# Filling half of the first expert's slots from the token groups already routed, and computing their products among the routing of the last group

## The chip, the cores and the metric

The kernel runs on 1 core of one Trainium2 chip. The metric is the time of one execution on the device, in microseconds (us), as the median over runs.

## What is computed

A linear attention with a decay per head, a gated MLP, and a mixture of experts in which each token goes to one expert:

```python
def reference(**kwargs):
    attn_out = _attn_ref(**attn_kwargs)                    # 2 x 8 heads x 768 x 64
    x = np.ascontiguousarray(attn_out.transpose(0, 2, 1, 3)).reshape(B * S, H * D)   # 1536 x 512
    x = _moe_ref(x=x, **moe_kwargs)       # silu(x @ w_gate) * (x @ w_val) @ w_out, d_ff 1536
    return _moe2_ref(x=x, **moe2_kwargs)

def _moe2_ref(x, w_gate, w1, w2):         # N 1536, D 512, E 8, F 1024
    logits = x @ w_gate
    expert_idx = np.argmax(logits, axis=1)
    probs = softmax(logits)
    for e in range(E):
        mask = expert_idx == e
        h = np.maximum(x[mask] @ w1[e], 0.0)
        out[mask] = gate_w[mask, None] * (h @ w2[e])
```

## The kernel before

Every product of the MLP and of the experts is made from float32 operands that are split in a high and a low part (fp32r), with three terms (`split_terms`): high times high, high times low, low times high. ScalarE (ACT) makes the high parts by a copy, VectorE (DVE) the low parts by a subtraction (helper `low`, L976 to L979).

**Attention**, 12 chunks of 128 tokens (`scores` L537, `from_state` L550, `to_state` L559, `within` L575), in plain f32.

**MLP**, three groups (`NG`) of 512 tokens, each with 12 units f (`NF1`) of 128 hidden columns. For each unit TensorE makes gate and val (`gate_val` L603, 24 products of 512 columns) and later the out products (`out_product` L618, 12 products, which wait for `hl`). gate_val of unit f+1 stands ahead of out_product of unit f. ACT and DVE have for each unit a function `unit` (L858, L1097): sigmoid, product, split of the next unit's weights, then `hid`, `hh`, `hl`. `first_half` holds units 0 to 5 and, spread among them, the routing of the group before; `second_half` units 6 to 11. In the last group's second half the weights of expert 0 are also loaded by GpSimd (POOL, `load_chunk` L420, eight halves of four pieces through `stage[2]`) and split (`split_first_expert`).

**Routing** of a group: the output is evacuated from PSUM in high and low part (`evacuate`), `logit_product` (L629, 8 products of 512 columns), DVE's `copy_logits`, `turn_logits` (four small transposes), `rows` (L651, four transposes for each of four tiles, which bring tokens onto partitions), ACT's `rows_out`, a store of each tile to `x2_rows` in DRAM. DVE's `choose` (L1130) finds the expert of each token, TensorE's `ranks` (L663) its rank among the tokens of that expert from the counts in `before`, `find_slots` and `place_tokens` (L1149, L1168) turn it to a slot, and `count_choices` adds the group to `before`. For the last group all this stands behind the MLP, and then a table: 12 small products (L722) give for each slot its token, DVE writes it as `idx`, and one product of `before` with ones counts the tokens of each expert, from which `passes` follows (one pass takes up to `CAP` = 256 tokens of each expert; slots go in token order). Two bursts of products that nothing reads, `keep_clock` (L658, 8 and 18 of them), stand in this stretch:

```python
            ranks(NG - 1)
            pe.wait_ge(ewl_ready, 1)
            keep_clock(8)
            for t in range(NT):          # the table, 12 products
            ...
            keep_clock(18)
            pe.wait_ge(idx_ready, 1)
            pe.wait_ge(slots_ready, 1)
```

**Experts.** POOL gathers the 256 rows of an expert by indirect DMA in two tiles `gx[0]`, `gx[1]` (`gather` L448), after it has waited for the stores of all rows. `transpose_rows` (L730) turns them (two times four transposes), ACT and DVE split them (`tokens`). Each expert then has 8 steps f: `hidden` (L739, 12 products of 256 columns, weights 128x128), ACT's Relu to `ehh` and DVE's low part `ehl`, `outward` (L752, 2 tiles x 3 products of 512 columns, which wait for `ehl`). Hidden f+1 stands ahead of outward f. Meanwhile the weights of the next expert are split, its rows transposed at f = 4, and its softmax factors made. `ys` is scaled by the gate and scattered by POOL. `read_passes` (L273) loads the number of passes to a register on each engine, ahead of expert 0. Experts 0 to 5 are a loop of two, then 6, then `last_expert`.

The order of the work on each engine is the order in which it is written. Buffers of the MLP and of the experts share memory (`region2`), as do routing tables and `stage[3]` (`region0`), so that e.g. the second expert's weights may be written only when the MLP's operands have been read.

Of the kernel before, what the change touches and what calls it, by code (L numbers as in the profile page):

```python
# [65 lines left out]
def bass_linear_attention_mlp_moe(nc, attn_in, lam_rows, mlp_w, router_w, expert_w, out):  # L66
    ctx = ExitStack()
    with ctx:
# [17 lines left out]
        idx_now = [sb(f"idx_now{i}", [P, 1], I32) for i in range(4)]  # L86
        gate_now = [sb(f"gate_now{i}", [P, 2]) for i in range(2)]
# [18 lines left out]
        mosti = sb("mosti", [P, 1], I32, region0)  # L106
        region0.close()
# [46 lines left out]
        lt = sb("lt", [2 * E, GT], F32, region2)  # L154
        region2.close()
# [77 lines left out]
        gate_ready_x = sem("gate_ready_x")  # L233
        gx_read = sem("gx_read")

# [32 lines left out]
        TOKEN_BANK, COUNT_BANK = 4, 5  # L268
# [18 lines left out]
        def _(sp):  # L287
# [46 lines left out]
            sp.wait_ge(gx_read, 4)  # L334
# [13 lines left out]
        def _(pool):  # L348
# [78 lines left out]
            with pool.Fori(1, PIECES) as q:  # L427
                for j in range(2):
                    pool.wait_ge(ewl_ready, q * 2 + (j - 1))
                    load_chunk(q, j)  # L430

            pool.wait_ge(rows_psum, NT)
            for i in range(2):
                nc.gpsimd.memset(gx[i][:, :], 0.0).then_inc(gx_read, 1)
            for t in range(GTT):
                pool.wait_ge(x2_stored[t], 16 * NG)

            def copy_idx(x, par):
                for i in range(2):
                    nc.gpsimd.tensor_copy(idx_now[2 * par + i][:, :],  # L440
                                          idx[:, bass.ds(x * 2 + i, 1)]).then_inc(now_ready, 1)

            def fetch(dst, src, at, done):
                nc.gpsimd.indirect_dma_start(
                    out=dst[:, :], out_offset=None, in_=src, in_offset=bass.IndirectOffsetOnAxis(ap=at, axis=0),
                    bounds_check=N - 1, oob_is_err=False).then_inc(done, 16)

            def gather(x):  # L448
                pool.wait_ge(gx_read, x * 2 + 2)
# [16 lines left out]
            def first_pass():  # L466
                gather(0)
                nc.gpsimd.memset(idx_now[0][:, :], 0).then_inc(now_ready, 2 * E)
# [8 lines left out]
            def gather_by_copy(x, par):  # L477

                pool.wait_ge(gx_read, x * 2 + 2)
# [3 lines left out]
                pool.wait_ge(now_ready, x * 2 + 2)  # L483
                for i in range(2):
                    fetch(gx[i], x2_rows, idx_now[2 * par + i][:, 0:1], gx_landed[i])

            def scatter_by_copy(x, par):
                for i, ready in ((0, y0_ready), (1, y1_ready)):
                    pool.wait_ge(idx_ready, 1)
                    pool.wait_ge(ready, x + 1)  # L490
                    put(i, idx_now[2 * par + i][:, 0:1])
# [28 lines left out]
            def ahead():  # L520
                pool.wait_ge(now_ready, 2 * E)
# [12 lines left out]
        def _(pe):  # L534
# [123 lines left out]
            def keep_clock(count):  # L658

                for _ in range(count):  # L660
                    mm(bank[:, ROWS_BANK, :], ewh0[:, 0, 0:P], ewh0[:, 0, KD * P:], start=True, stop=True)

# [29 lines left out]

            def second_half(g, end=False):
# [17 lines left out]
            second_half(NG - 1, end=True)  # L711
            logit_product(NG - 1)
            before_turn(NG - 1)
            turn_logits()
            pe.wait_ge(x2f_ready, NG * KD)
            for t in range(GTT):
# [5 lines left out]
            for t in range(NT):  # L722
                pe.wait_ge(places_ready, t + 1)
                last = mm(bank[:, TOKEN_BANK, 0:NCOLS], place[:, t, :], token_at[:, t, :],
                          start=(t == 0), stop=(t == NT - 1))
            last.then_inc(table_psum, 1)
            pe.wait_ge(before_ready, NG + 1)
            mm(bank[:, COUNT_BANK, 0:E], ones[:, :], before[:, :], start=True, stop=True).then_inc(table_psum, 1)

            def transpose_rows(x):  # L730
                for i in range(2):
                    pe.wait_ge(gx_landed[i], (x + 1) * 16)
                    pe.wait_ge(exl_ready, x * 2)
                    for k in range(KD):
# [39 lines left out]

            def outward_tile(x, f, t):
# [40 lines left out]
        def _(act):  # L816
# [41 lines left out]
            def unit(g, f, following, chunks=()):  # L858
# [7 lines left out]
                for c in chunks:  # L866
                    split_first_expert(c)
                act.wait_ge(hid_ready, u + 1)
# [33 lines left out]
            def second_half(g, end=False):  # L902
                for f in range(HALF, NF1):
                    unit(g, f, (g, f + 1) if f < NF1 - 1 else None if end else (g + 1, 0),
                         FIRST_CHUNKS[f - HALF] if end else ())
# [5 lines left out]
            second_half(NG - 1, end=True)  # L911
            evacuate(NG - 1)
            for t in range(GTT):
                rows_out(NG - 1, t, t)
            def tokens(x, par):
                for i in range(2):
                    act.wait_ge(gx_read, x * 2 + i + 3)
# [8 lines left out]
            def expert(x, par, more):  # L926
                for f in range(NF2):
# [3 lines left out]
                    if more:  # L931
                        split_expert(1 - par, f, f // 2, expert_loads(x + 1, f // 2))
                        if f == 5:
# [5 lines left out]
                                     scale=gate_now[par][:, 0:1]).then_inc(y0_ready, 1)  # L939

            def last_expert(x):
                for f in range(NF2):
# [7 lines left out]
                                     scale=gate_now[1][:, 0:1]).then_inc(y0_ready, 1)  # L950
# [3 lines left out]
                                     scale=gate_now[1][:, 1:2]).then_inc(y1_ready, 1)  # L954

            def experts(base, first):
                if not first:
                    for f in range(NF2):
                        split_expert(0, f, f // 2, expert_loads(base, f // 2))
# [6 lines left out]

            n = read_passes(act)
            experts(0, True)
            further_passes(act, n, lambda p: experts(p * E, False))
# [3 lines left out]
        def _(dve):  # L973
# [222 lines left out]

            def second_half(g, end=False):
                for f in range(HALF, NF1):
                    unit(g, f, (g, f + 1) if f < NF1 - 1 else None if end else (g + 1, 0),
                         FIRST_CHUNKS[f - HALF] if end else ())  # L1200
# [5 lines left out]
            second_half(NG - 1, end=True)  # L1206
            evacuate(NG - 1)
# [16 lines left out]
            V.tensor_scalar(idx[:, :], bank[:, TOKEN_BANK, 0:NCOLS], float(EMPTY), None, ALU.add).then_inc(idx_ready, 1)  # L1224
# [5 lines left out]

            def tokens(x, par):
                for i in range(2):
                    low(exl[par][:, :, i * P:(i + 1) * P], bank[:, T_BANK + i, :].rearrange("p (k i) -> p k i", k=KD),
                        exh[par][:, :, i * P:(i + 1) * P], exh_ready, x * 2 + i + 1, exl_ready)
                dve.wait_ge(expo_ready, x + 1)
# [4 lines left out]
                V.reciprocal(gate_now[par][:, :], den_eps[:, :]).then_inc(gate_ready_x, 1)  # L1240

            def expert(x, par, more):
# [12 lines left out]
                V.tensor_scalar(ys[1][:, :], bank[:, Y_BANK + 1, 0:DM], gate_now[par][:, 1:2], None,  # L1255
# [9 lines left out]
            def experts(base, first):  # L1265
                if not first:
                    for f in range(NF2):
# [50 lines left out]
```

## Time and profile before

| | |
|---|---|
| median of 3 runs | 568.12 us (567.39 to 568.15) |
| the profiled execution | 568.24 us, of which its span in the trace is 566.5 |
| mean granted TensorE clock | 0.99 |
| busy: TensorE / VectorE / ScalarE / GpSimd | 548.6 / 320.8 / 230.8 / 77.2 us |
| attention, MLP, routing of the last group and wait, experts | to about 60 us, to 353.6, to 372.3, to the end |

PE is the row of TensorE's matmuls and PEld that of its weight loads, which overlap them; the end of a matmul in the records lies behind the start of the next, since they are pipelined, so a price per product is read from start to start. "Granted clock" 1.00 is 2.4 GHz and 0.50 is 1.2 GHz. Times inside the trace count from the start of the span.

### The profile page before, as it was taken

What the parts mean: (1) busy time and instruction counts of PE and PEld (TensorE: products, weight loads), DVE (VectorE), ACT (ScalarE), POOL (GpSimd) and SP (SyncE); (2) the same over time, 40 slices, a digit from 0 to 9 for tenths busy, and PEclk for the clock granted to TensorE, in tenths of its full rate; (3) what the DMA queues carried; (4) which work ended last, traced back from release to release, by engine and by line L of the source; (5) the groups of instructions that cost most, each with busy time, mean ns of one, the idle gap of its engine ahead of it and who ended that gap; (6) DMA issues with size and microseconds to landing.
All of it is one profiled execution on the core that took longest, in us unless ns stands there. A gap on an engine that the chain in (4) does not pass through costs nothing. (4 is left out here: it accounts for less than half of the span.)

```text
span 566.5 us, 8798 instructions
## 1 busy us (share of the span) xinstructions
PE 548.6 (97%) x3290; PEld 467.4 (83%) x3290; DVE 320.8 (57%) x540; ACT 230.8 (41%) x377; POOL 77.2 (14%) x94
## 2 busy tenths in 40 slices
PE   7999999999999999999999999889999999999994
PEld 6888888888878888887888888579999999999983
DVE  7777544544655544545556665546666766766620
ACT  3114332332443432335434543345555554655510
POOL 5972000000000000000000010211130321312001
PEclk9999999999999999999999999979999999999998
DMA  8886433123313243223154555235665756654000
GB/s 299 310 284 201 156 111 111 63 107 111 108 60 126 79 150 111 72 95 111 56 149 139 179 167 222 95 118 208 225 233 186 258 192 235 219 171 184 2 26 34
DMA packets 18432, 84.45 MB, mean 149 GB/s; under 512 B 3036, under 2 KB 3036, under 8 KB 14816
## 3 DMA queue, kind: packets, MB, share of 16 engines
q1 hardware_dynamic: 13536, 71.35, 36.6%
q0 software_dynamic: 3712, 10.54, 5.4%
q10 hardware_dynamic: 1152, 2.13, 1.0%
q8 instruction: 20, 0.33, 0.2%
q14 instruction: 12, 0.10, 0.0%
HBM read 78.73 MB, written 7.39 MB: 152 GB/s over the span
## 5 line engine op out<-in xcount | busy, mean ns | idle before, releaser
L979 DVE TENSOR_TENSOR ewl<-stage,ewh 128x1024 fp32r<-128x1024 f32 x64 | 78.0, 1222 | 23.0 <-ACT ewh L818 23.0
L1100 DVE TENSOR_TENSOR sig<-bank,sig 128x512 f32<-128x512 f32 x36 | 24.9, 692 | 99.4 <-ACT sig L863 99.4
L613 PE MATMUL bank<-xh,gvh 128*128 (+1 forms) x288 | 77.1, 389 | 0.0
L613 PE MATMUL bank<-xh,gvl 128*128 (+1 forms) x288 | 77.0, 389 | 0.0
L613 PE MATMUL bank<-xl,gvh 128*128 (+1 forms) x288 | 77.0, 389 | 0.0
L818 ACT ACTIVATE ewh<-stage 128x1024 fp32r<-128x1024 f32 x64 | 67.0, 1052 | 0.9 <-DMA stage<-expert_w 0.9
L863 ACT ACTIVATE sig<-bank 128x512 f32<-128x512 f32 x36 | 21.7, 602 | 104.7 <-PE bank L613 104.7
L613 PEld LDWEIGHTS bank<-xh,gvh 128*128 128x128 f32 x288 | 54.0, 188 | 11.3 <-issue 0.2
L613 PEld LDWEIGHTS bank<-xh,gvl 128*128 128x128 f32 x288 | 54.1, 188 | 11.2
L613 PEld LDWEIGHTS bank<-xl,gvh 128*128 128x128 f32 x288 | 54.1, 188 | 11.2
L623 PE MATMUL bank<-hh,woh 128*128 128x512 f32 x144 | 56.8, 395 | 0.0
L623 PE MATMUL bank<-hh,wol 128*128 128x512 f32 x144 | 56.1, 390 | 0.0
L623 PE MATMUL bank<-hl,woh 128*128 128x512 f32 x144 | 56.1, 390 | 0.0
L818 ACT ACTIVATE hh<-hid 128x512 fp32r<-128x512 f32 x36 | 22.8, 632 | 76.5 <-DVE hid L1109 76.5
L929 ACT ACTIVATE ehh<-bank 128x256 fp32r<-128x256 f32 x56 | 21.6, 385 | 69.6 <-PE bank L746 69.4
L1064 DVE TENSOR_TENSOR gvl<-stage,gvh 128x1024 fp32r<-128x1024 f32 x36 | 44.1, 1226 | 8.8 <-ACT gvh L818 8.8
L756 PE MATMUL bank<-ewl,ehh 128*128 128x512 f32 x112 | 44.1, 394 | 0.0
L756 PE MATMUL bank<-ewh,ehl 128*128 128x512 f32 x112 | 44.0, 393 | 0.0
L756 PE MATMUL bank<-ewh,ehh 128*128 128x512 f32 x112 | 43.8, 391 | 0.0
L746 PE MATMUL bank<-exh,ewh 128*128 128x256 f32 x256 | 42.1, 288 | 1.5 <-DVE exl L979 1.5
L746 PEld LDWEIGHTS bank<-exh,ewh 128*128 128x128 f32 x256 | 38.7, 193 | 5.8 <-issue 1.7
L423 POOL DMA_DIRECT2D stage<-expert_w x8 | 4.5, 566 | 278.9 <-DVE ewl L979 278.4
(145 smaller groups left out, 846.9 us busy)
## 6 DMA issues: line engine op xcount, KB each, us to landing
stage<-expert_w SPq DMA_DIRECT2D x28, 1024.0 KB, 4.9
stage<-mlp_w SPq DMA_DIRECT2D x36, 768.0 KB, 4.4
stage<-attn_in SPq DMA_DIRECT2D x24, 512.0 KB, 5.3
stage<-expert_w POOLq DMA_DIRECT2D x8, 512.0 KB, 5.6
x_rows<-x ACTq DMA_DIRECT2D x8, 260.0 KB, 5.1
x_rows<-x SPq DMA_DIRECT2D x4, 260.0 KB, 4.2
gx<-x_rows,idx POOLq DMA_INDIRECT x16, 4.6
out<-ys,idx POOLq DMA_INDIRECT x16, 3.9
```

The lines of the kernel that those rows point to most:

```text
L423: pool.dma_start(stage[2][:, half], expert_w[0, q][:, half]).then_inc(first_landed[j], 16)
L613: last = mm(bank[:, where, :], wt[:, k, :], (xh, xl)[x][:, k, bass.ds(g * GT, GT)], start=(at == 0), stop=(at == 3 * KD - 1))
L623: last = mm(bank[:, d, :], (woh, wol)[w][f % 3][:, d * P:(d + 1) * P], (hh, hl)[x][f % 2][:, :], start=(f == 0 and n == 0), stop=True, ski ...
L746: last = mm(bank[:, H_BANK + f % 2, 0:CAP], expert_bufs(par)[w][:, f, k * P:(k + 1) * P], (exh, exl)[z][par][:, k, :], start=(at == 0), st ...
L756: last = mm(bank[:, Y_BANK + t, 0:DM], (ehh, ehl)[z][f % 2][:, t * P:(t + 1) * P], expert_bufs(par)[w][:, f, KD * P:], start=(f == 0 and n ...
L818: return nc.scalar.activation(dst, src, ACT.Copy)
L863: nc.scalar.activation(sig[:, :], bank[:, GATE_BANK, :], ACT.Sigmoid).then_inc(sig_ready, 1)
L929: nc.scalar.activation(ehh[f % 2][:, :], bank[:, H_BANK + f % 2, 0:CAP], ACT.Relu).then_inc(ehh_ready, 1)
L979: V.tensor_tensor(dst, src, high.bitcast(F32), ALU.subtract).then_inc(inc, 1)
L1064: V.tensor_tensor(gvl[f % 2][:, :], stage[f % 2][:, 0:GV], gvh[f % 2][:, :].bitcast(F32), ALU.subtract).then_inc(gvl_ready, 1)
L1100: V.tensor_tensor(sig[:, :], bank[:, GATE_BANK, :], sig[:, :], ALU.mult).then_inc(sg_ready, 1)
```

## The change

Expert 0's 256 slots become two tiles of 128. Tile A holds the first 128 tokens of expert 0, which have to come from groups 0 and 1. In the last MLP group, at unit 6, TensorE makes a table from the first two groups alone (`table_a`, 8 small products, and a count of `before`), DVE turns it into `idx_a` and adds to expert 0's count in `before` what it lacks to 128 (`slots_a`), POOL gathers tile A between its weight chunks (`gather_a`), TensorE transposes it between gate_val of unit 11 and out_product of unit 10 (`transpose_a`), and in unit 11 ACT and DVE split it to `exa`, ahead of their `hid`, `hh` and `hl` (`rows_a`).

Behind the MLP both bursts of `keep_clock` go. Hidden and outward products of tile A (12 products of 128 columns and 3 of 512 for each f) stand among the parts of the routing of group 2 and behind them. The table of all groups comes after `hidden_a(3)`; tile B is gathered alone (`gather_b`) and transposed after `outward_a(5)`. Then follows tile B of expert 0 (`first_expert`), again 12 products of 128 and 3 of 512 columns for each f, with the transposes for expert 1 at f = 5. ACT and DVE split expert 1's weights during tile A and the first three f of tile B instead of during expert 0. `read_passes` goes behind expert 1; expert 1 is written out, experts 2 to 5 are the loop. SP's load of the last quarter of expert 1's weights waits for the landing of tile B's gather instead of four marks of `gx_read`, which included the memsets of `gx`; those move into `gather_a` and `gather_b`. `idx_now` and `gate_now` become one tensor each.

```diff
@@ gpsimd
-            with pool.Fori(1, PIECES) as q:
-            pool.wait_ge(rows_psum, NT)
-            for i in range(2):
-                nc.gpsimd.memset(gx[i][:, :], 0.0).then_inc(gx_read, 1)
+            def gather_a():
+                pool.wait_ge(lt_psum, NG - 1)
+                nc.gpsimd.memset(gx[0][:, :], 0.0).then_inc(gx_zero, 1)
+                pool.wait_ge(idx_a_ready, 1)
+                for t in range(GTT):
+                    pool.wait_ge(x2_stored[t], 16 * (NG - 1))
+                pool.wait_ge(gx_zero, 1)
+                fetch(gx[0], x2_rows[0:(NG - 1) * GT, :], idx_a[:, 0:1], gx_landed[0], (NG - 1) * GT)
+            next_chunks(1)
+            next_chunks(2)
+            gather_a()
+            next_chunks(3)
+            def gather_b():
+                pool.wait_ge(val_ready, NG * NF1)
+                nc.gpsimd.memset(gx[1][:, :], 0.0).then_inc(gx_zero, 1)
...
+                fetch(gx[1], x2_rows, idx[:, 1:2], gx_landed[1])
@@ tensor
-            def keep_clock(count):
+            def table_a():
+                pe.wait_ge(places_ready, (NG - 1) * GTT)
+                pe.wait_ge(before_ready, NG)
+                nt = (NG - 1) * GTT
+                for t in range(nt):
+                    mm(bank[:, ROUTE_BANK, TABLE_COL:TABLE_COL + NCOL], place[:, t, :], token_at[:, t, 0:NCOL],
+                       start=(t == 0), stop=(t == nt - 1))
+                mm(bank[:, ROUTE_BANK, COUNT_COL:COUNT_COL + E], ones[:, :], before[:, :],
+                   start=True, stop=True).then_inc(table_a_psum, 1)
@@ second_half
+                    if end and f == HALF:
+                        table_a()
+                    if end and f == NF1 - 2:
+                        transpose_a()
                     out_product(g, f)
@@ behind the MLP
+            def hidden_a(f):
+                pe.wait_ge(exl_ready, 1)
+                pe.wait_ge(ewl_ready, f + 1)
+                if f >= 2:
+                    pe.wait_ge(eal_ready, f - 1)
...
+                        last = mm(bank[:, H_BANK + f % 2, 0:P], expert_bufs(0)[w][:, f, k * P:(k + 1) * P],
+                                  exa[z][:, k, :], start=(at == 0), stop=(at == 3 * KD - 1))
...
+            pe.wait_ge(exl_ready, 1)
             logit_product(NG - 1)
-            before_turn(NG - 1)
+            hidden_a(0)
+            pe.wait_ge(lt_ready, NG)
+            pe.wait_ge(before_ready, NG + 1)
             turn_logits()
             pe.wait_ge(x2f_ready, NG * KD)
-            for t in range(GTT):
+            for t in range(GTT - 1):
                 rows(NG - 1, t, t)
             ranks(NG - 1)
-            pe.wait_ge(ewl_ready, 1)
-            keep_clock(8)
+            rows(NG - 1, GTT - 1, GTT - 1)
+            hidden_a(1)
+            for f in range(2):
+                outward_a(f)
+                hidden_a(f + 2)
+            table()
+            for f in range(2, NF2 - 3):
+                outward_a(f)
+                hidden_a(f + 2)
+            outward_a(NF2 - 3)
+            transpose_b()
+            hidden_a(NF2 - 1)
+            outward_a(NF2 - 2)
+            outward_a(NF2 - 1)
...
-            keep_clock(18)
-            pe.wait_ge(idx_ready, 1)
-            pe.wait_ge(slots_ready, 1)
             pe.wait_ge(rows_ready, NT)
+            first_expert()
+            expert(1, 1, True)
             n = read_passes(pe)
-            experts(0)
@@ scalar
+            def rows_a():
+                act.wait_ge(gx_read, 1)
+                copy(logits_a[:, :], gx[0][:, DM:])
+                copy(exa[0][:, :, :], bank[:, A_BANK, :].rearrange("p (k i) -> p k i", k=KD)).then_inc(exh_ready, 1)
...
             evacuate(NG - 1)
+            relu_a(0)
             for t in range(GTT):
                 rows_out(NG - 1, t, t)
+            relu_a(1)
+            for f in range(2, NF2 - 1):
+                relu_a(f)
+                split_second_expert(f - 2)
+            rows_b()
+            relu_a(NF2 - 1)
+            split_second_expert(NF2 - 3)
+            nc.scalar.activation(expo[:, 0, :], logits_a[:, :], ACT.Exp)
+            nc.scalar.activation(expo[:, 1, :], gx[1][:, DM:], ACT.Exp).then_inc(expo_ready, 1)
@@ vector
             choose(NG - 1)
+            low_a(0)
             find_slots(NG - 1)
+            low_a(1)
             place_tokens(NG - 1)
+            low_a(2)
+            dve.wait_ge(before_ready, NG + 1)
             count_choices(NG - 1, more=False)
...
+            for f in range(3, NF2):
+                low_a(f)
+                split_second_expert(f - 3)
+                if f == NF2 - 2:
+                    low(exl[0][:, :, P:], bank[:, ROUTE_BANK, :].rearrange("p (k i) -> p k i", k=KD),
+                        exh[0][:, :, P:], exh_ready, 2, exl_ready)
```

## Rows read from the trace of the kernel before

**Rows 1.** The page, part 1: busy us, share of the span, instructions of each engine.
```profile
PE 548.6 (97%) x3290; PEld 467.4 (83%) x3290; DVE 320.8 (57%) x540; ACT 230.8 (41%) x377; POOL 77.2 (14%) x94
```

**Rows 2.** Stretches: busy us and instructions of each engine, granted clock, DMA share, GB/s.
```profile
353.60:372.30 18.70, 13.50 (x81) 9.14 (x79) 9.01 (x36) 6.73 (x13) 3.22 (x5) 0.97 0.28 86
372.30:376.00 3.70, 3.66 (x17) 3.66 (x18) 0.78 (x4) 1.49 (x5) 1.75 (x2) 0.50 0.77 285
```

**Rows 3.** Chain that ended last, in order of time: start, us, what.
```profile
398.21 2.75 PE bank L746 x24
400.96 1.37 PE bank L756 x6
...
410.61 0.87 PE bank L735 x8
...
421.19 2.75 PE bank L746 x24
```

**Rows 4.** Timeline of TensorE, starts of gate_val in groups 1 and 2.
```profile
248.45 1.07 PE L613 MATMUL bank<-xh,gvh 128*128 x4
...
256.61 1.07 PE L613 MATMUL bank<-xh,gvh 128*128 x4
...
284.61 1.07 PE L613 MATMUL bank<-xh,gvh 128*128 x4
...
293.27 1.07 PE L613 MATMUL bank<-xh,gvh 128*128 x4
```

**Rows 5.** Timeline, last unit of the MLP.
```profile
348.36 0.69 DVE L1109 TENSOR_TENSOR hid<-bank,sig 128x512 f32<-128x512 f32 x1 [1.40 <-PE bank L613]
...
349.75 0.69 DVE L979 TENSOR_TENSOR hl<-hid,hh 128x512 fp32r<-128x512 f32 x1 [0.70 <-ACT hh L818]
...
350.88 0.39 PE L623 MATMUL bank<-hh,woh 128*128 128x512 f32 x1
...
353.37 0.39 PE L623 MATMUL bank<-hh,wol 128*128 128x512 f32 x1
```

**Rows 6.** Timeline, routing of the last group to the first hidden product.
```profile
354.69 1.08 PE L636 MATMUL bank<-xl,router_hl 128*16 128x512 f32 x4
...
358.16 0.19 DVE L1147 TENSOR_TENSOR ohb<-rt,rv 128x32 bf16<-128x32 f32 x1
358.27 1.82 SPq L331 DMA_DIRECT2D x_rows<-x  x4
...
360.75 0.37 PEld L724 LDWEIGHTS bank<-token_at,place 128*128 128x128 f16 x8 [0.26 <-issue]
...
362.78 0.26 DVE L1224 TENSOR_SCALAR idx<-bank 128x96 int32<-128x96 f32 x1
...
362.87 4.39 PE L661 MATMUL bank<-ewh 128*128 128x512 f32 x18
...
365.28 1.08 POOL L444 DMA_INDIRECT gx<-x_rows,idx  x1 [5.36 <-issue]
...
368.74 0.66 PE L735 MATMUL bank<-ident,gx 128*128 128x128 f32 x4 [1.48 <-DMA gx<-x_rows,idx]
...
370.06 0.69 DVE L979 TENSOR_TENSOR exl<-bank,exh 128x512 fp32r<-128x512 f32 x1 [6.47 <-ACT exh L818]
...
372.34 1.22 PE L746 MATMUL bank<-exh,ewh 128*128 128x256 f32 x4 [1.49 <-DVE exl L979]
```

**Rows 7.** Groups of weight loads: line, weights, shapes, count, busy us, mean ns.
```profile
L746 PEld LDWEIGHTS bank<-exh,ewh 128*128 128x128 f32 x256 | 38.7, 193 | 5.8 <-issue 1.7
...
L571 PEld LDWEIGHTS bank<-stage,kd 128*64 128x64 f32 x160 | 5.5, 137 | 1.9 <-ACT kd L847 0.9
...
L636 PEld LDWEIGHTS bank<-xh,router_hl 128*16 128x16 f32 x12 | 1.1, 94 | 1.7 <-ACT xh L818 0.5
```

**Rows 8.** Timeline of TensorE's weight loads in the attention, plain f32, 128 columns.
```profile
33.92 0.97 PEld L555 LDWEIGHTS bank<-qs,state 128*128 128x128 f32 x8 [0.17 <-issue]
```

**Rows 9.** Stretches, the attention; columns as in Rows 2.
```profile
14.00:50.00 36.00, 35.55 (x510) 30.93 (x507) 27.23 (x48) 7.55 (x12) 26.36 (x25) 1.00 0.83 281
```

More of the change, by code:

```diff
@@ L106, in bass_linear_attention_mlp_moe @@
         mosti = sb("mosti", [P, 1], I32, region0)
+        idx_a = sb("idx_a", [P, 1], I32, region0)
+        lack, lift = [sb(f"lift{i}", [P, 1], F32, region0) for i in range(2)]
         region0.close()
@@ L154, in bass_linear_attention_mlp_moe @@
         lt = sb("lt", [2 * E, GT], F32, region2)
+        exa = [sb(f"exa{i}", [P, KD, P], F32R, region2) for i in range(2)]
         region2.close()
@@ L520, in ahead @@
             def ahead():
[L521 removed]
+                pool.wait_ge(now_ready, 2 * E - 2)
                 all_stored(E)
@@ new lines, in outward_a, with table @@
+            def outward_a(f):
+                pe.wait_ge(eal_ready, f + 1)
+                for n, (w, z) in enumerate(split_terms):
+                    last = mm(bank[:, A_BANK, 0:DM], (ehh, ehl)[z][f % 2][:, 0:P], expert_bufs(0)[w][:, f, KD * P:],
+                              start=(f == 0 and n == 0), stop=(f == NF2 - 1 and n == 2))
+                if f == NF2 - 1:
+                    last.then_inc(y_psum, 1)
+            def table():
+                pe.wait_ge(route, (NG - 1) * STEPS + 6)
+                for t in range(NT):
+                    pe.wait_ge(places_ready, t + 1)
+                    last = mm(bank[:, ROUTE_BANK, TABLE_COL:TABLE_COL + NCOLS], place[:, t, :], token_at[:, t, :],
+                              start=(t == 0), stop=(t == NT - 1))
+                last.then_inc(table_psum, 1)
+                pe.wait_ge(before_ready, NG + 2)
+                pe.wait_ge(rows_ready, (NG - 1) * GTT + 1)
+                mm(bank[:, COUNT_BANK, 0:E], ones[:, :], before[:, :],
+                   start=True, stop=True).then_inc(table_psum, 1)
@@ L712, in _, with transpose_b @@
+            def transpose_b():
+                pe.wait_ge(slots_ready, 1)
+                pe.wait_ge(gx_landed[1], 16)
+                for k in range(KD):
+                    last = nc.tensor.transpose(bank[:, ROUTE_BANK, k * P:(k + 1) * P], gx[1][:, k * P:(k + 1) * P],
+                                               ident[:, :])
+                last.then_inc(gx_read, 1)
+            pe.wait_ge(exl_ready, 1)
             logit_product(NG - 1)
-            before_turn(NG - 1)
+            hidden_a(0)
@@ L733, in transpose_rows @@
                     pe.wait_ge(exl_ready, x * 2)
+                    if first and i:
+                        pe.wait_ge(y0_ready, 1)
                     for k in range(KD):
@@ L856, in _, with unit @@
             split_mlp(0, 1)
-            def unit(g, f, following, chunks=()):
+            def unit(g, f, following, chunks=(), between=None):
                 u = g * NF1 + f
@@ L953, in last_expert, with experts @@
                 nc.scalar.activation(ys[1][:, :], bank[:, Y_BANK + 1, 0:DM], ACT.Copy,
[L954 to L959, printed above, removed]
+                                     scale=gate_now[:, 1, 1:2]).then_inc(y1_ready, 1)
+            def experts(base):
+                for f in range(NF2):
+                    split_expert(0, f, f // 2, expert_loads(base, f // 2))
                 tokens(base, 0)
@@ L965, in experts @@
                 last_expert(base + (E - 1))
+            first_expert()
+            expert(1, 1, True)
             n = read_passes(act)
-            experts(0, True)
-            further_passes(act, n, lambda p: experts(p * E, False))
+            with act.Fori(1, E // 2 - 1) as i:
+                for par in range(2):
+                    expert(i * 2 + par, par, True)
+            expert(E - 2, 0, True)
+            last_expert(E - 1)
+            further_passes(act, n, lambda p: experts(p * E))
         @block.vector
@@ L1263, in last_expert, with experts @@
                                            op1=ALU.subtract).then_inc(ehl_ready, 1)
-            def experts(base, first):
-                if not first:
-                    for f in range(NF2):
-                        split_expert(0, base, f, f // 2)
+            def experts(base):
+                for f in range(NF2):
+                    split_expert(0, base, f, f // 2)
                 tokens(base, 0)
```

196 lines of the change are left out of this document (155 added, 41 removed).

## The prediction

> **What bounds the kernel now.** I read the busy times first: TensorE is busy 97% of the span [rows 1], so it is the bound nearly everywhere and only stretches where it waits, or works at less than full clock, can be won. The view of stretches shows the one such place: from 353.6 to 372.3 us it has 13.50 us of recorded work, part of it filler (`keep_clock`), and at 372.3 the granted clock is 0.50, the lower level of 1.2 GHz [rows 2]. The chain in order of time then gives the price of an undisturbed expert: expert 1 runs from 398.21 to 421.19, 22.98 us, in which 24 hidden products of 256 columns take 2.75 us (0.1145 each), six outward products of 512 columns 1.37 (0.229 each), eight transposes 0.87 [rows 3]. Expert 0 starts at 372.34 [rows 6] and so takes 25.87, 2.9 more, which is the half clock. The last MLP product begins at 353.37 and passes to the next 0.23 later, at 353.60 [rows 5]; I call that T. Expert 1 now starts at T + 44.6.
>
> The change puts tile A of expert 0 (128 slots) into this gap, and tile B behind it. It must be gained between T and the start of expert 1; what follows is untouched and full of TensorE work.
>
> **1. The last MLP group gets longer.** A unit without extras lasts 8.16 us (248.45 to 256.61), one with four transposes 8.66 (284.61 to 293.27): four transposes cost 0.50 [rows 4]. `transpose_a` is such a four. `table_a` adds nine small products; eight loads of the same kind take 0.37 us, 0.04 each, so about 0.3 to 0.4 [rows 6]. Its DVE part, `slots_a`, four small operations in unit 7, lies in slack. `rows_a` does not. In the last unit VectorE starts `hid` at 348.36 and ends `hl` at 349.75 + 0.69 = 350.44; the last out product starts at 350.88, just without a wait [rows 5]. Now DVE must first make the low part of tile A: transposes, ACT copy and DVE subtract took from 368.74 to 370.75, 2.0 us [rows 6], plus some 0.2 for the copy of the logits. Beginning at about 348.2, this ends at 350.4, `hid` starts 2.1 late, `hl` ends near 352.5, and the product starts near 352.75 instead of 350.88: 1.9 late, of which 0.5 are the transposes. With `table_a` the group ends **2.2 us later**. Bounds: 0.8 if `hl` were hidden, 3 if two more semaphore steps count.
>
> Tile A's gather is no stall: POOL issues it after the third pair of weight chunks, about 20 us ahead of `transpose_a`; issue to use took 365.28 to 368.74, 3.5 us [rows 6]. The last chunks are issued about 2 us later than before, in a stage that has a unit (8.16) to spare. SP now waits for one landing in place of four reads; what is queued behind it is the last quarter of expert 1's weights, needed only in tile B.
>
> **2. The price of a narrow product.** Tile A and tile B each need per f 12 hidden products of 128 columns, a shape in fp32r that the trace of before lacks. Bounds: 0.057 (half of the 256-wide one, streaming alone) and 0.22 (below). I take **0.1145**, the price of the 256-wide, because the weight load doesn't shrink: its duration is 94 ns for 16 columns of weights, 137 for 64 and 193 for 128 [rows 7], i.e. (193-94)/112 = 0.88 ns a column, 113 ns for 128 columns over a fixed part that overlaps. A load that takes 0.11 us behind a stream of 0.053 sets the pace. The nearest narrow row agrees: eight loads of plain f32 at 128 columns in 0.97 us, (0.97-0.19)/7 = 0.111 [rows 8]. Hence halving the tile saves nothing on hidden products, only on outward ones (three for six): per f 12 x 0.1145 + 3 x 0.229 = 2.06, per tile 16.5, two tiles 33.0, against 22.1 for the expert whole. So 10.9 us are added, to be paid out of 44.6 - 23.0 = 21.6 us of routing, filler, wait and low clock.
>
> The Trainium skill, TensorE: Matmul & The Clock Gate, section "Back-to-back issue gap", speaks for another price: about 81 ns per matmul at 128 columns in a stream of loads and matmuls. By it the sum would be 192 x 33.5 ns = 6.4 us lower, 559.7. No row here shows such a pace for f32 weights.
>
> **3. T' to the end of tile A** (T' = T + 2.2). TensorE's own work: logits 2.2 (353.6 to 354.69 + 1.08, [rows 6]), turned logits 0.4 (four at 0.1), 16 transposes 2.0 by part 1, 18 small products of ranks, table and count 0.7, tile A 16.5, `transpose_b` 0.5: 22.3.
>
> Waits between, followed through the queues: `hidden_a(0)` puts `choose` 0.5 later than now (`ohb` at 358.16, [rows 6]), hidden by it. ACT turns to `relu_a(1)` only after the four row copies, so VectorE places tokens about 1.2 later than now; the table comes after `hidden_a(3)`, at T' + 12.3; `idx` is ready at 12.7 (now 362.78 + 0.26 - 353.6 = 9.4, [rows 6]). The gather was in fact issued 2.2 after `idx`, at 365.28, since POOL waits for the row stores issued from 358.27 on [rows 6]; those are only 1 later, and so landed by 12.7. So tile B's rows can be used at 12.8 + 3.5 = 16.3, while TensorE reaches `transpose_b` at about 19: three us of margin. Low parts of A: every `low_a(f)` has the 2.06 of one f against DVE's 0.3 + 1.2 for its own part and a quarter-piece split; only `low_a(7)` can't be covered: `hidden_a(7)`, Relu, subtract, load against 0.69 of outward work: 0.35. Sum **22.7**.
>
> **4. Tile B to expert 1.** 16.5, the transposes for expert 1 0.87, the same uncovered end 0.35: **17.7**. ACT's table load, two exps and the gates of A come before VectorE's first low of B, which needs them only one hidden product later; covered. If that cover fails, at most 1 us. `read_passes` moves from the gap to behind expert 1, on PE, ACT and DVE. No row shows it. It lay between the end of TensorE's filler (362.87 + 4.39 = 367.26) and 368.74 [rows 6], so it costs 0 to 1.5; the outward products queued ahead of it are 1.37, and ACT and DVE have as much slack there: I take 0. GpSimd's two memsets were off the path.
>
> **Sum.** 2.2 + 22.7 + 17.7 = 42.6 instead of 44.6: 2.0 faster. The profiled execution took 568.24 (span 566.5 and 1.7 around it), 0.12 above the median; so 566.2 against it, and **566.1** as median. A measurement of this kernel can tell about 0.2% (1.1 us) from no change. The own range of this case is 564.0 to 568.5, from the bounds of parts 1 and 4.
>
> **Rivals.**
> *A. The narrow product costs more than the wide one: slower.* Plain f32 of 128 columns takes two instructions for each product here, 0.111 each [rows 8], 0.22 together. If an fp32r product this narrow is done no faster, each of the 192 costs 0.106 more: 20.3 more, 586.4. It decides early: 2.0/192 = 0.0104, so from a pitch of **0.125** on the gain is gone, and from 0.131 the kernel is measurably slower. For it: no row shows an fp32r product below 256 columns. Against it: one instruction per product, and a load that explains 0.1145 without it. Chance 0.16, a quarter of it with prices up to 0.155 (574).
> *B. The clock.* The filler that held it is gone; what stands there waits 1.3 us before the last out product and then streams only half of the time. If it is granted 1.2 GHz as at 372.3 [rows 2], a loss like expert 0's 2.9 comes back: 569.1; over a longer stretch, more. Against it: the attention's narrow products ran at clock 1.00 [rows 9]. Chance 0.14, up to 574.
> *C. Narrow products are cheap.* At 0.057 the two tiles save 11.0, but then `transpose_b` would come at 14.4 and wait until 16.3: 9.1 gained over the forecast, 557.0. Chance 0.06, with the page's price in it.
> That the lift makes a further pass is excluded: on the reference's inputs expert 0 has 79 + 67 = 146 tokens in groups 0 and 1 and 220 in all, so nothing is lifted, and no expert passes 256.
>
> **The numbers.** Forecast 0.64, A 0.16, B 0.14, C 0.06. Of the forecast's own case 7 in 10 lie below 567.0, 2 in 10 within 0.2%. Faster 0.64 x 0.7 + 0.06 = 0.51; same 0.13 + 0.05 of the mild B = 0.18; slower the rest, 0.31. The range leaves out A's expensive three quarters (0.12) and C (0.06): 562 to 574.
>
> **What would show it.** Narrow hidden products at 0.114 to 0.116 of start-to-start in tiles A and B; the last MLP product 2.2 later; one wait of 1.3 on `hl` before it; the table near T' + 12, no wait of PE on the gather; clock 1.00 throughout; expert 1 starting at 396.2. It is wrong if the pitch is over 0.125, if the clock row is under 1.00 between T' and there, or if PE waits on DVE's low parts of A in more than the last place.

## The result and the profile after

The changed kernel takes 565.62 us (median of 6 runs, 564.96 to 566.59) against 568.13 (6 runs, 567.39 to 568.56): ratio 0.9958, interval 0.9945 to 0.9971, 2.5 us faster. Run again beside the last experiments (`after_again`) it took 565.73 (11 runs) against 567.80, ratio 0.9964 (0.9953 to 0.9976), 2.1 us faster. 566.1 was forecast. All times and ratios are those of fast runs; only one run of all, 573.3 us in `e3_three_moves`, was not fast, and it is left out below.

| | before | after |
|---|---|---|
| median | 568.13 | 565.62 |
| profiled execution, its span | 568.24, 566.5 | 566.59, 564.9 |
| busy TensorE / VectorE / ScalarE / GpSimd | 548.6 / 320.8 / 230.8 / 77.2 | 551.9 / 321.1 / 232.2 / 80.0 |
| first hidden product of expert 1 | 398.05 | 395.78 |

TensorE is busy 3.3 us longer in a span that is 1.6 shorter. The chain that ended last, of the changed kernel, in order of time (start, us, what; L653 out products of the MLP, L666 logits, L769 and L777 tile A's hidden and outward products, L786 the table, L798 `transpose_b`, L883 and L896 tile B's, L845 and L855 those of the whole experts), answers to [rows 3]:

```profile
353.42 3.01 PE bank L653 x12
356.43 2.01 PE bank L666 x8
358.45 1.29 PE bank L769 x12
...
367.68 0.53 PE bank L786 x12
...
375.11 0.44 PE bank L798 x4
375.55 1.29 PE bank L769 x12
376.84 1.65 PE bank L777 x6
378.49 2.63 PE bank L883 x24
...
385.91 1.29 PE bank L883 x12
387.20 0.74 PE bank L896 x3
...
395.94 2.73 PE bank L845 x24
...
418.90 2.75 PE bank L845 x24
```

It is TensorE's own work nearly without a break. One f of a tile is 1.29 + 0.74 = 2.03 us. Twelve narrow products take 1.29, 0.1075 each, against 1.38 for twelve wide ones (2.75 / 2). But the three outward products behind them take 0.74 instead of 0.69, so the whole f says more: (2.03 - 0.69) / 12 = 0.112 for a narrow product. The stretches of the same kernel (columns as in [rows 2]) answer to [rows 2]: the granted clock is 1.00 where it was 0.50.

```profile
350.00:356.00 6.00, 5.28 (x23) 4.05 (x22) 2.93 (x5) 2.70 (x6) 0.09 (x1) 1.00 0.19 79
...
370.00:375.00 5.00, 5.00 (x37) 4.56 (x37) 3.41 (x7) 3.05 (x6) 1.33 (x2) 1.00 0.26 51
375.00:380.00 5.00, 5.00 (x39) 4.45 (x38) 3.47 (x7) 4.18 (x8) 0.00 (x0) 1.00 0.94 382
380.00:385.00 5.00, 5.00 (x40) 4.75 (x40) 3.79 (x8) 3.23 (x6) 3.63 (x2) 1.00 0.99 369
```

Between 345 and 400 us the only wait of TensorE's products over 0.5 us stands ahead of the last out products. The timeline of the changed kernel there answers to [rows 5] (L733 is `transpose_a`, L1158 the low parts):

```profile
349.33 0.60 PE L733 MATMUL bank<-ident,gx 128*128 128x128 f32 x4
...
350.69 0.69 DVE L1158 TENSOR_TENSOR exa<-bank,exa 128x512 fp32r<-128x512 f32 x1 [2.56 <-ACT exa L947]
...
351.30 0.68 DVE L1288 TENSOR_TENSOR hid<-bank,sig 128x512 f32<-128x512 f32 x1
...
352.68 0.69 DVE L1158 TENSOR_TENSOR hl<-hid,hh 128x512 fp32r<-128x512 f32 x1 [0.70 <-ACT hh L947]
...
353.42 0.50 PE L653 MATMUL bank<-hh,woh 128*128 128x512 f32 x1 [0.72 <-DVE hl L1158]
```

`hid` waits for `exa`'s low part, `hl` for `hid`, and TensorE for `hl`.

**A difference ahead of the change.** This profiled execution is the slowest of its six runs, and part of that lies in the attention, whose instructions the change doesn't touch. Stretches 7 to 14 us, before and then after:

```profile
7.00:14.00 7.00, 4.96 (x95) 4.57 (x96) 6.40 (x12) 3.87 (x14) 2.46 (x3) 1.00 1.01 399
```

```profile
7.00:14.00 7.00, 5.28 (x76) 4.83 (x74) 5.83 (x11) 3.77 (x14) 2.66 (x3) 0.76 1.01 393
```

For some 3 us the clock was granted at half, and the MLP runs 0.8 us late from then on (the gate_val of unit 5 in group 2 starts at 302.73 instead of 301.92). The row is 0.76 in `after_again` too, and in four traces of the variants below (`e2_rows_behind`, `e3_three_moves`, `e7_logits_b`, `e8_load_later`); it is 1.00 in those of the other four (`e4_wide`, `e5_half_width`, `e6_twice`, `e9_two_moves`), of the kernel before and of `e1_filler`. With 0.76 that gate_val starts between 302.28 and 302.99, with 1.00 between 301.41 and 301.92. So it is no fixed part of the changed kernel, but whether the change makes it likelier isn't shown: only two traces have the old order. The steps are therefore compared from start to start below.

**A second trace.** `after_again` was expected to take 565.2 to 566.0, and to start expert 1 near 395.0 if the attention had the full clock. It took 565.73; the clock was 0.76 again, and expert 1 starts at 395.33, in its timeline:

```profile
395.33 0.62 PE L845 MATMUL bank<-exh,ewh 128*128 128x256 f32 x4
```

Its gate_val of group 2 starts at 302.28, 0.36 late. Counted from there both traces agree: 93.05 us to expert 1, where the kernel before needs 96.13, so the change gains 3.08 us in this stretch.

### The profile page after: what moved, and what is told of

It reads as the page before. It is cut to its first block, busy times and chain, and to the rows that moved or that the text cites. A ratio compares the mean times of both kernels' runs of the same rounds, so it can differ in the third digit from the quotient of the medians.

```text
span 564.9 us, 8870 instructions
## 1 busy us (share of the span) xinstructions
PE 551.9 (98%) x3369; PEld 472.5 (84%) x3369; DVE 321.1 (57%) x552; ACT 232.2 (41%) x386; POOL 80.0 (14%) x94
## 4 chain that ended last, share of the span: by engine, by line
PE 95%; DVE 1%; ACT 1%; issue 0%; DMA 0%; POOL 0%; POOLq 0%
PE bank L643 35%; PE bank L653 17%; PE bank L845 14%; PE bank L855 12%; PE bank L612 2%; PE bank L576 2%; PE bank L585 2%; PE bank L903 2%; PE bank L769 2%; PE bank L883 2%; PE bank L601 1%; PE bank L777 1%; PE bank L834 1%; PE bank L684 1%; PE bank L666 1%; PE bank L896 1%
## 5 line engine op out<-in xcount | busy, mean ns | idle before, releaser
L1158 DVE TENSOR_TENSOR ewl<-stage,ewh 128x1024 fp32r<-128x1024 f32 x64 | 78.0, 1222 | 20.0 <-ACT ewh L947 20.0
L653 PE MATMUL bank<-hh,woh 128*128 128x512 f32 x144 | 57.2, 397 | 0.7 <-DVE hl L1158 0.7
L653 PE MATMUL bank<-hh,wol 128*128 128x512 f32 x144 | 56.2, 390 | 0.0
L653 PE MATMUL bank<-hl,woh 128*128 128x512 f32 x144 | 56.2, 390 | 0.0
L947 ACT ACTIVATE hh<-hid 128x512 fp32r<-128x512 f32 x36 | 22.7, 632 | 75.7 <-DVE hid L1288 75.7
L1103 ACT ACTIVATE ehh<-bank 128x256 fp32r<-128x256 f32 x48 | 18.5, 385 | 59.6 <-PE bank L845 59.4
L1158 DVE TENSOR_TENSOR hl<-hid,hh 128x512 fp32r<-128x512 f32 x36 | 24.9, 693 | 25.1 <-ACT hh L947 25.1
L446 POOL DMA_INDIRECT gx<-x_rows,idx x15 | 22.1, 1475 | 114.7 <-issue 95.4
L947 ACT ACTIVATE gvh<-stage 128x1024 fp32r<-128x1024 f32 x36 | 38.1, 1057 | 0.0
L855 PE MATMUL bank<-ewl,ehh 128*128 128x512 f32 x96 | 37.9, 394 | 0.0
L855 PE MATMUL bank<-ewh,ehl 128*128 128x512 f32 x96 | 37.7, 393 | 0.0
```

The lines of the kernel that those rows point to most:

```text
L446: nc.gpsimd.indirect_dma_start(out=dst[:, :], out_offset=None, in_=src, in_offset=bass.IndirectOffsetOnAxis(ap=at, axis=0), bounds_check=c ...
L653: last = mm(bank[:, d, :], (woh, wol)[w][f % 3][:, d * P:(d + 1) * P], (hh, hl)[x][f % 2][:, :], start=(f == 0 and n == 0), stop=True, ski ...
L855: last = mm(bank[:, Y_BANK + t, 0:DM], (ehh, ehl)[z][f % 2][:, t * P:(t + 1) * P], expert_bufs(par)[w][:, f, KD * P:], start=(f == 0 and n ...
L947: return nc.scalar.activation(dst, src, ACT.Copy)
L1103: nc.scalar.activation(ehh[f % 2][:, :], bank[:, H_BANK + f % 2, 0:CAP], ACT.Relu).then_inc(ehh_ready, 1)
L1158: V.tensor_tensor(dst, src, high.bitcast(F32), ALU.subtract).then_inc(inc, 1)
```

## Experiments

Each ran beside the kernel before; `e4_wide` and `e5_half_width` on another chip than the others. "The changed kernel" is 565.7.

**Is it the packing or the clock?** `e1_filler` is the kernel before with more filler and nothing moved (bank 5 is read by nobody there):

```diff
-            def keep_clock(count):
+            def keep_clock(count, where=7):
...
-                    mm(bank[:, ROWS_BANK, :], ewh0[:, 0, 0:P], ...)
+                    mm(bank[:, where, :], ewh0[:, 0, 0:P], ...)
@@ transpose_rows, for expert 0
                     last.then_inc(gx_read, 1)
+                    if fill:
+                        keep_clock((4, 7)[i], 5)
@@
-            keep_clock(18)
+            keep_clock(24)
```

> The kernel before, with TensorE kept busy through the gap by 6 more filler products of 512 columns ahead of the wait for the gather, 4 behind the first gathered tile's transposes and 7 behind the second's. Nothing is moved into the gap. Theory K (the clock): expert 0's half-clocked start goes, 25.87 falls to 23.0 us, and the kernel gains 2.9 minus at most 0.3 for filler that runs over: 565.2 to 565.5, as fast as the change. Rival P (the packing brings the gain, a granted clock at this place doesn't hang on filler): the clock still falls at 372 us and the time stays within 0.5 of 568.1.

Measured: 565.69 (565.50 to 567.18) against 568.32, ratio 0.996 (0.9946 to 0.9973): 2.6 us faster, as much as the whole change. Its timeline of TensorE and then its stretch at the start of expert 0:

```profile
368.97 0.65 PE L735 MATMUL bank<-ident,gx 128*128 128x128 f32 x4 [0.38 <-DMA gx<-x_rows,idx]
369.38 1.18 PE L661 MATMUL bank<-ewh 128*128 128x512 f32 x4
370.39 0.60 PE L735 MATMUL bank<-ident,gx 128*128 128x128 f32 x4
370.75 1.86 PE L661 MATMUL bank<-ewh 128*128 128x512 f32 x7
372.49 0.74 PE L748 MATMUL bank<-exh,ewh 128*128 128x256 f32 x4
```

```profile
372.30:376.00 3.70, 3.70 (x29) 3.42 (x28) 1.45 (x6) 2.74 (x7) 1.60 (x2) 1.00 0.72 279
```

Expert 0 starts 0.15 later than before, at full clock, and expert 1 starts at 395.51 (the chain gives 395.67 for its first 24): expert 0 takes 23.0 instead of 25.7. Theory K holds and P falls. So the 2.7 us of the low clock were what there was to win cheaply, and 17 more products that nobody reads (6, 4 and 7) win them. What the packing adds is the difference of the two from T on: expert 1 starts at T + 41.9 with filler and, as is worked out below, at T + 41.4 with the change.

**The price of a narrow product.** `e6_twice` issues each hidden product of tile B twice:

```diff
-                            last = mm(bank[:, H_BANK + f % 2, 0:P], expert_bufs(0)[w][:, f, k * P:(k + 1) * P],
-                                      (exh, exl)[z][0][:, k, P:], start=(at == 0), stop=(at == 3 * KD - 1))
-                            at += 1
+                            for _ in range(2):
+                                last = mm(..., start=(at == 0), stop=(at == 6 * KD - 1))
+                                at += 1
```

> The changed kernel with every hidden product of tile B issued twice (96 more products of 128 columns; the hidden values double, so the output is that of another function). Nothing but TensorE has more work. Theory L (the load of 128 columns of weights sets the pace): 96 x 0.111 = 10.7 us more. Rival S (streaming alone, 0.053 each, the rest is switching between hidden and outward work): 5.1 us more. Rival F (the price of plain f32, 0.22): 21 us more.

Measured: 575.95 (575.66 to 576.22), 10.3 us over the changed kernel: 0.107 for each of the 96. By the ratios to the kernel before (1.0134 against 0.9958) it is 10.0. In its chain 24 narrow products in a row take 2.63, and one f lasts 3.37 instead of 2.03, 0.112 for each product more:

```profile
386.32 0.74 PE bank L898 x3
387.06 2.63 PE bank L884 x24
```

`e4_wide` makes tile B's products 256 columns wide, `e5_half_width` 64:

```diff
-  ... bank[:, H_BANK + f % 2, 0:P] ... (exh, exl)[z][0][:, k, P:]
+  ... bank[:, H_BANK + f % 2, 0:2 * P] (as 2 x 128) ... (exh, exl)[z][0][:, k:k + 1, P:].broadcast_to([P, 2, P])   # e4_wide
+  ... bank[:, H_BANK + f % 2, 0:P // 2] ... (exh, exl)[z][0][:, k, P:P + P // 2]                                # e5_half_width
```

> The changed kernel, with tile B's 96 hidden products reading their 128 columns twice over, so that each streams 256 columns (the second 128 results are read by nobody). Theory L (the load of 128 columns of weights sets the pace of a narrow product): from 0.1085 to 0.1145 us per product, 0.3 to 0.7 us more in all. Rival S (streaming sets it): 96 x 0.053 = 5.1 us more.

> The changed kernel, with tile B's 96 hidden products on 64 of its 128 columns only (half of tile B's hidden values are left out, so its output is not computed). Theory L: the load keeps its length, and the time stays within 0.5 us of the changed kernel. Rival S: 96 x 0.027 = 2.6 us less.

Measured: 566.09 (565.57 to 566.75) wide and 565.22 (564.89 to 565.55) at half width, so four times the columns cost 0.9 us over 96 products. Within the traces it is plainer. Timelines of TensorE, `e4_wide` first:

```profile
384.78 0.64 PE L883 MATMUL bank<-exh,ewh 128*128 128x256 f32 x4
385.26 0.62 PE L883 MATMUL bank<-exl,ewh 128*128 128x256 f32 x4
```

```profile
384.85 0.61 PE L883 MATMUL bank<-exl,ewh 128*128 128x64 f32 x4
385.30 0.61 PE L883 MATMUL bank<-exh,ewl 128*128 128x64 f32 x4
```

Four products of 256 columns take 0.48, four of 64 take 0.45 (0.1125 each), like the changed kernel's of 128. A whole f, from one first product to the next, lasts 2.07 at 256 columns, 2.03 at 128 and 2.04 at 64: between 64 and 256 columns the price hardly depends on the width. S and F fall, and the price is fixed, as theory L has it. That it is the load of the weights, and not another fixed cost of a product of this type, rests on [rows 7] and isn't shown; no run here varied the columns of weights.

**The late `hl`.** `e2_rows_behind` moves tile A's split behind `hh` and `hl`:

```diff
@@ scalar, unit
-                if between:
-                    between()
                 act.wait_ge(hid_ready, u + 1)
                 copy(hh[f % 2][:, :], hid[:, :]).then_inc(hh_ready, 1)
+                if between:
+                    between()
@@ vector, unit
                 low(hl[f % 2][:, :], hid[:, :], hh[f % 2][:, :], hh_ready, u + 1, hl_ready)
+                if behind:
+                    behind()
```

> The changed kernel, with tile A's split in high and low part moved behind hh and hl of the last unit on ACT and DVE. Theory Q (hl is late because the split stands ahead of it): TensorE's wait of 0.72 us ahead of the last out products goes, hid starts 1.8 us earlier, and with the exposed first load the last MLP group ends about 0.8 to 1.0 earlier; 0.8 to 1.0 us faster than the changed kernel. Rival R: the split then delays the evacuation or the first hidden product by as much, and the sum stays within 0.3 of the changed kernel.

Measured: 564.32 (564.07 to 565.46) against 568.32, ratio 0.9929 (0.9916 to 0.9941), 1.4 under the changed kernel. In its timeline `hid` starts at 349.32 instead of 351.30, 1.8 earlier if the 0.2 from ahead are taken off. The split, now behind, still ends at 352.0, long before tile A's first product (357.07):

```profile
349.32 0.69 DVE L1288 TENSOR_TENSOR hid<-bank,sig 128x512 f32<-128x512 f32 x1 [1.40 <-PE bank L643]
...
350.71 0.69 DVE L1158 TENSOR_TENSOR hl<-hid,hh 128x512 fp32r<-128x512 f32 x1 [0.70 <-ACT hh L947]
...
351.31 0.68 DVE L1158 TENSOR_TENSOR exa<-bank,exa 128x512 fp32r<-128x512 f32 x1
```

TensorE's wait ahead of the last out products is gone, and the logits start 1.0 us earlier, counted from the gate_val of group 2 (52.53 us behind it instead of 53.54). Theory Q holds; R falls. Not all of it arrives in this trace: expert 1 starts only 0.24 earlier, since TensorE now waits for expert 1's second tile of rows. In its timeline:

```profile
389.74 0.66 PE L834 MATMUL bank<-ident,gx 128*128 128x128 f32 x4 [0.59 <-DMA gx<-x_rows,idx]
```

This execution, 565.46, is the slowest of its five. That the median gains 1.4, more than the 0.8 to 1.0 of the theory, no trace explains.

**Two more waits, and what they uncovered.** `e3_three_moves` adds to it the first hidden products of tile B between the last two outward steps of tile A, and takes the transposes and splits for expert 1 one f forward; `e9_two_moves` has the first of these two alone.

```diff
             outward_a(NF2 - 2)
+            hidden_b(0)
             outward_a(NF2 - 1)
@@ first_expert, PE; and f == 6 to f == 5 for tokens(1, 1) on ACT and DVE     # e3_three_moves only
-                    if f == 5:
+                    if f == 4:
                         transpose_rows(1, True)
```

> The same move as e2_rows_behind, and two more: the first hidden products of tile B stand between the last two outward steps of tile A (covers the wait on the last low part of A), and the transposes and splits for expert 1 come one f earlier in tile B (so that DVE's last low part of B is not queued behind them). Theory: each of the two waits of 0.4 and 0.5 us of the trace goes, 0.6 to 0.8 us faster than e2_rows_behind. Rival: the waits only move to the next outward step or to the gather of expert 1's rows, and the time equals that of e2_rows_behind within 0.3.

> e2_rows_behind with only the first hidden products of tile B moved between the last two outward steps of tile A; the transposes for expert 1 stay at f = 5. Theory: the wait of 0.4 us at the end of tile A goes but TensorE comes to expert 1's rows as much earlier and waits there: within 0.3 us of e2_rows_behind. Rival: 0.4 faster than e2_rows_behind.

Measured: 565.16 (564.19 to 566.39), ratio 0.9942 (0.9927 to 0.9957), and 564.57 (563.69 to 569.33), ratio 0.9947 (0.9929 to 0.9966). The theory of `e3_three_moves` failed: it is not faster than `e2_rows_behind` (0.9929), and its median is 0.8 higher, though the intervals overlap. It had mis-sized the waits: 0.4 and 0.5 us are what the weight loads wait, while the products of the changed kernel come only 0.2 and 0.3 late. The median of `e9_two_moves` is within 0.3 of `e2_rows_behind`, as its theory has it, but by the ratios it is 1.0 us slower; the two can't be told apart. Its runs spread over 5.6 us, those of the changed kernel over 1.6. The timeline of `e3_three_moves`, POOL's issues and TensorE's transposes:

```profile
379.54 1.98 POOL L446 DMA_INDIRECT gx<-x_rows,idx  x1 [9.24 <-issue]
...
381.83 1.50 POOL L446 DMA_INDIRECT gx<-x_rows,idx  x1 [0.30 <-issue]
...
387.20 0.66 PE L850 MATMUL bank<-ident,gx 128*128 128x128 f32 x4 [0.51 <-DMA gx<-x_rows,idx]
388.35 0.66 PE L850 MATMUL bank<-ident,gx 128*128 128x128 f32 x4 [0.49 <-DMA gx<-x_rows,idx]
```

Expert 1's rows take 7.7 and 6.5 us from issue to use, where 3.5 was the price in the kernel before [rows 6]. The profiled execution of `e9_two_moves`, 569.33, is its longest and shows what a late gather can cost, in its timeline and then its stretches:

```profile
390.33 0.66 PE L850 MATMUL bank<-ident,gx 128*128 128x128 f32 x4 [2.24 <-DMA gx<-x_rows,idx]
```

```profile
386.00:392.00 6.00, 3.76 (x31) 3.35 (x30) 0.29 (x1) 0.28 (x1) 0.00 (x0) 1.00 0.42 163
392.00:398.00 6.00, 6.00 (x24) 5.24 (x24) 2.29 (x7) 1.72 (x6) 2.78 (x3) 0.53 0.19 51
```

One late gather, landed 8.8 us after issue, makes TensorE wait 2.2 us, and the clock falls to 0.53 behind it: rival B's loss came, in a variant. The other runs above the median left no trace, so whether they have the same cause isn't shown. Two kernels test where the lateness is from. In `e7_logits_b` ACT copies tile B's logits away behind `transpose_b`, so that POOL gathers expert 1's rows 4 us earlier; in `e8_load_later` SP holds the weights of expert 2 back until the rows are there.

```diff
@@ e7_logits_b: scalar, rows_b; POOL's gather(1) waits for logits_b_ready instead of expo_ready
+                copy(logits_b[:, :], gx[1][:, DM:]).then_inc(logits_b_ready, 1)
@@ e8_load_later: sync
             n = read_passes(sp)
+            for i in range(2):
+                sp.wait_ge(gx_landed[i], 32)
             with sp.Fori(2, E) as e:
```

> e3_three_moves, and ACT copies tile B's eight logits out of gx[1] right behind tile B's transposes, so that POOL may gather expert 1's rows then, some 4 us earlier than behind the exps of expert 0's gates. Theory G (in e3_three_moves TensorE waits 1.0 us for expert 1's rows, whose gather takes 7 us beside 4 MB of weights for expert 2): the wait goes, 1.0 us faster than e3_three_moves, about 564.3 where that is 565.3. Rival H (e3_three_moves is slow by the scatter of its runs): equal to it within 0.4.

> e3_three_moves, with SP's loads of expert 2's weights held back until expert 1's rows have landed; nothing else. Theory G: issue to landing of expert 1's two gathers falls from over 6 us to about 3.5, TensorE's wait of 1.0 us on them goes, and the time is that of e7_logits_b within 0.4. Rival I (the gather is slow on POOL's own side, 1.5 to 2.0 us for an issue instead of 1.0): the durations of the issues stay and with them at least half of the wait.

Measured: 563.78 (563.33 to 564.78), ratio 0.9929 (0.9914 to 0.9945), and 564.15 (563.68 to 564.51), 0.9935 (0.992 to 0.995), both against 567.80. TensorE waits for no gather in either. Counted from the gate_val of group 2, expert 1 starts after 91.69 us in `e7_logits_b` and 91.73 in `e8_load_later`, after 93.14 in `e3_three_moves`: 1.4 less. The times alone wouldn't exclude rival H, since the intervals of their ratios overlap with that of `e3_three_moves`; the traces do. The stretch 376 to 388 us of `e3_three_moves` and then of `e8_load_later`, and the latter's timelines:

```profile
376.00:388.00 12.00, 11.35 (x82) 10.05 (x80) 6.60 (x13) 6.41 (x13) 3.48 (x2) 1.00 0.99 355
```

```profile
376.00:388.00 12.00, 12.00 (x94) 11.33 (x92) 6.35 (x13) 6.00 (x12) 3.48 (x2) 1.00 0.27 83
```

```profile
379.14 1.98 POOL L448 DMA_INDIRECT gx<-x_rows,idx  x1 [9.24 <-issue]
381.42 1.50 POOL L448 DMA_INDIRECT gx<-x_rows,idx  x1 [0.30 <-issue]
...
386.13 1.03 PE L852 MATMUL bank<-ident,gx 128*128 128x128 f32 x8
```

POOL's issues are as long as in `e3_three_moves` (rival I falls), but with the DMA engines 27% busy instead of 99% they land 3.2 to 4.4 us after issue and nothing waits. Theory G holds: the gather collided with expert 2's weights. The change brought the two together from both sides. Timelines of POOL and of SP's queue, before and then after:

```profile
373.95 1.00 POOL L444 DMA_INDIRECT gx<-x_rows,idx  x1 [6.15 <-issue]
380.62 17.97 SPq L321 DMA_DIRECT2D stage<-expert_w  x4
```

```profile
375.06 11.11 SPq L334 DMA_DIRECT2D stage<-expert_w  x4
380.57 1.97 POOL L446 DMA_INDIRECT gx<-x_rows,idx  x1 [9.23 <-issue]
```

The weights start 5.6 us earlier, because expert 1's are split earlier, and the gather 6.6 us later, because it has to wait until tile B's logits are read. What was issued 6.7 us ahead of the weights now comes 5.5 us behind them. `e8_load_later` undoes the first, `e7_logits_b` part of the second (375.87, with the DMA engines 97% busy), and either is enough. `e7_logits_b`, the fastest kernel here, is 1.95 under the changed one beside it, and 4.0 under the kernel before.

## Why the prediction was right

The range, the sign and the size held: 2.0 forecast, 2.5 measured. The mechanism held too, but that the numbers are so near is in part luck: its three terms were 1.2 us too high together, and 0.4 to 0.8 us lost ahead of them and 0.2 behind them, which it didn't forecast, hid 0.5 to 1.0 of it. The steps, one by one:

- **The last MLP group, 2.2.** From gate_val in group 2 to the logits the group got 1.86 longer: 0.35 by `table_a` (gate_val of unit 7 starts at 319.40 instead of 318.24, 1.16 late, of which 0.81 are from the attention), 1.51 by the rest (356.27 instead of 353.60, 2.67 late). `hid` was 1.8 late, not 2.1, the wait for `hl` 0.7, not 1.3, and four transposes behind gate_val took 0.35, not 0.50. The mechanism was right; `e2_rows_behind` shows that its larger part was avoidable.
- **The narrow product, 0.1145.** 0.112 by the whole f, 0.1075 over twelve by themselves; the first four after an outward step take only 0.40. That is just under the 0.114 to 0.116 that were to show it. Right; a price by streaming (rival C) or of plain f32 (rival A) is excluded by the three runs that change the count or the width. The Trainium skill's figure of about 81 ns at 128 columns (TensorE: Matmul & The Clock Gate, "Back-to-back issue gap") doesn't hold for this type of weights: the traces say 107 to 112.
- **Tile A with the routing, 22.7.** 356.27 to 378.32 is 22.05, the difference being partly 8 x 0.03 and shorter small products (12 of the table in 0.53). `idx` was ready at 368.50, T' + 12.2 (12.7 forecast), and tile B's rows were there at `transpose_b`. For the last low part the weight load waited 0.4, which made the products 0.2 late (0.35 forecast).
- **Tile B, 17.7.** 378.32 to 395.78 is 17.46.
- **The sum.** 1.86 + 22.05 + 17.46 = 41.4 after T, instead of 44.45 (398.05 less 353.60): 3.1 gained, 2.0 forecast. The forecast's 44.6 took expert 1's start from the chain (398.21) and expert 0's from the timeline (372.34). Both from the timeline, expert 0 takes 25.7, and the low clock cost 2.7, not 2.9. The first profiled execution starts expert 1 only 2.27 earlier, because it was 0.8 late ahead of the change. `after_again` closes the account: 3.08 gained, 0.36 lost ahead, 0.16 lost in the experts behind (five take 114.90 instead of 114.72 in the first trace), and its span is 2.5 shorter, like its time. In the first trace the end behind the last scatter's issue is 0.4 longer than in the other two, and so the span only 1.6 shorter; why is open.
- **`read_passes`, 0.** Expert 2 starts 22.96 after expert 1, where before it was 22.98. Right.
- **Rival B, the clock.** 1.00 through both tiles. The waits (0.7 us of the products, 0.4 and 0.5 of the weight loads) left it there; 2.2 us of waiting in `e9_two_moves` didn't.

What the prediction didn't see: it counted the low clock as 2.9 of the 21.6 us to pay from, and didn't say that filler alone would give nearly the whole gain; and it followed SP's last load to its end, but neither the loads behind it, which start earlier, nor expert 1's gather, which starts later and loses the room that it had. In the changed kernel the gather still comes in time: transposes at 389.80 with no wait.

## What to carry to other kernels

Before rebuilding a stage around an idle stretch, price what the pieces cost when cut: two tiles of 128 columns paid 10.4 us (16 x 2.03 against 22.1) because each narrow product costs nearly as much as a wide one. The useful work in the gap gave 0.5 more in the trace than 17 more filler products that kept the clock, and nothing that the medians tell apart. Look at the granted clock behind each wait first, since it was the cheapest thing to win here, and was lost again in the variant that waited 2.2 us. When an engine gets ahead, follow the loads that it frees on every queue, down to the small transfer that has to land among them.

## What the runs showed that was not expected

- An fp32r product with 128 columns of weights costs 0.11 us at 64, 128 and 256 moving columns.
- A gather of 128 rows takes 3.5 us from issue to use with the DMA engines 29% busy (the kernel before, 364 to 369 us) and 7.7 beside 4 MB of weights.
- POOL's issue of such a gather takes 1.0 to 1.1 us or 1.5 to 2.0, in the kernel before too (1.88 at 417.67). In the twelve traces each of the 88 longer issues begins while VectorE makes a low part `ewl` out of `stage` and `ewh`, and ends 0.9 us behind that instruction; none of the 104 shorter ones begins there. The timeline of the changed kernel has the issue at 380.57, shown above, beside this:

```profile
380.42 1.21 DVE L1158 TENSOR_TENSOR ewl<-stage,ewh 128x1024 fp32r<-128x1024 f32 x1
```

  No run moved the one against the other, so what makes it wait isn't shown.
